# Low parts of the first network's inner activations moved from GpSimd to VectorE for two chunks

## The reference

```python
# 1. causal mix over 7 taps, softmaxed per head (8 heads of 24 channels)
out = einsum('hk,bskhg->bshg', softmax(weight), windows_of_7(x))
# 2. first network, d_ff = 1536
g = x @ w_gate;  val = x @ w_val
x = (g * sigmoid(g) * val) @ w_out
# 3. second network, d_ff = 2048
h = x @ w_in
x = where(h > 0, h, exp(min(h, 0)) - 1) @ w_out
```

## Time and profile before

| | |
|---|---|
| median of 3 runs | 1205.99 us |
| the profiled execution | 1206.76 us |
| its span, first to last instruction | 1205.0 us |
| TensorE busy | 1199.5 us, 100% |
| VectorE / ScalarE / GpSimd busy | 775.5 / 664.2 / 717.9 us |
| stages: chunk 0 first network | 13.93 to 51.05 us |
| chunk 1 first network, second network | 51.05 to 90.14, 90.14 to 124.39 us |
| chunk 2 first network, second network | 124.39 to 165.73, 165.73 to 198.52 us |

### The profile page before, as it was taken

One profiled execution on the slowest core, in us unless ns is written; L12 is line 12 of the kernel. 1 busy time (PEld: TensorE's weight loads), 2 busy tenths in 40 slices (PEclk: granted clock), 3 DMA queues, 4 the chain that ended last, 5 costly groups with the idle time before them and its releaser, 6 DMA issues.

```text
span 1205.0 us, 31390 instructions
## 1 busy us (share of the span) xinstructions
PE 1199.5 (100%) x11798; PEld 1032.4 (86%) x11798; DVE 775.5 (64%) x1178; ACT 664.2 (55%) x1114; POOL 717.9 (60%) x528
## 2 busy tenths in 40 slices
PE   9999999999999999999999999999999999999999
PEld 7988888888888888889888898888988889888898
DVE  6787575675656756567665666656666476675665
ACT  6456555465554645546455464655546556465565
POOL 6787656574654746547465474654746557465565
PEclk9999999999999999999999999999999999999999
DMA  7412012120111211012110121100212002120110
GB/s 179 109 51 44 12 27 41 32 44 11 32 31 30 44 30 23 21 30 44 30 27 17 30 44 30 35 17 22 44 30 41 11 22 44 30 44 9 30 34 15
DMA packets 103955, 43.37 MB, mean 36 GB/s; under 512 B 75888, under 2 KB 93936, under 8 KB 103920
## 3 DMA queue, kind: packets, MB, share of 16 engines
q1 hardware_dynamic: 103104, 42.29, 15.7%
q10 hardware_dynamic: 816, 0.59, 0.2%
HBM read 16.12 MB, written 6.29 MB: 19 GB/s over the span
## 4 chain that ended last, share of the span: by engine, by line
PE 97%; POOL 1%; DVE 1%; issue 1%; ACT 0%; ACTq 0%; DVEq 0%
PE up L860 55%; PE down L860 42%; POOL hid_lo L441 1%; DVE mixed L830 0%; DVE act L771 0%; PE down L1063 0%; POOL up_w_lo L326 0%; DVE hidden L787 0%; ACT L617 0%; ACT hid_hi L608 0%; POOL y_main L445 0%; POOL halves L445 0%; DVE mixed L827 0%; DVE taps_head L813 0%; ACT act L593 0%
## 5 line engine op out<-in xcount | busy, mean ns | idle before, releaser
L441 POOL TENSOR_TENSOR hid_lo<-hidden,hid_hi 128x512 fp32r<-128x512 f32 x447 | 623.7, 1405 | 473.2 <-ACT hid_hi L574 304.8
L860 PE MATMUL down<-out_w,hid_hi 64*128 64x384 f32 x2040 | 300.4, 355 | 0.0
L734 DVE TENSOR_TENSOR hidden<-act,up 128x512 f32<-128x512 f32 x191 | 130.8, 685 | 249.1 <-ACT act L557 249.1
L860 PE MATMUL down<-out_w,hid_lo 64*128 64x192 f32 x2040 | 260.8, 251 | 0.3 <-POOL hid_lo L441 0.3
L771 DVE TENSOR_SCALAR act<-up 128x512 f32<-128x512 f32 x256 | 164.8, 685 | 112.0 <-PE up L860 112.0
L860 PE MATMUL up<-in_b_hi,up_w_hi 64*128 64x512 f32 x1128 | 224.1, 393 | 0.0
L860 PE MATMUL up<-in_b_hi,up_w_lo 64*128 64x512 f32 x1128 | 223.7, 393 | 0.0
L860 PE MATMUL up<-in_b_lo,up_w_hi 64*128 64x512 f32 x1128 | 223.6, 393 | 0.0
L574 ACT ACTIVATE hid_hi<-hidden 128x512 fp32r<-128x512 f32 x192 | 121.5, 633 | 177.9 <-DVE hidden L734 160.5
L608 ACT ACTIVATE hid_hi<-hidden 128x512 fp32r<-128x512 f32 x256 | 156.9, 628 | 96.5 <-DVE hidden L787 79.4
L593 ACT ACTIVATE act<-act 128x512 f32<-128x512 f32 x256 | 156.1, 631 | 94.8 <-DVE act L771 94.8
(11 more groups left out here) (96 smaller groups left out, 1085.9 us busy)
## 6 DMA issues: line engine op xcount, KB each, us to landing
x_raw<-x_dram SPq DMA_DIRECT2D x136, 64.0 KB, 2.2
out_dram<-stage SPq DMA_DIRECT2D x15, 384.0 KB, 2.7
in_b_hi<-in_b_hi SPq DMA_DIRECT2D x32, 128.0 KB, 2.3
in_b_lo<-in_b_lo SPq DMA_DIRECT2D x32, 128.0 KB, 2.3
swapped<-halves SPq DMA_DIRECT2D x32, 128.0 KB, 2.3
in_a_hi<-in_a_hi SPq DMA_DIRECT2D x30, 128.0 KB, 2.3
in_a_lo<-in_a_lo SPq DMA_DIRECT2D x30, 128.0 KB, 2.3
stage<-w_out_dram SPq DMA_DIRECT2D x7, 384.0 KB, 3.9
```

Source lines behind the costliest of these rows:

```text
L441: return pool.tensor_tensor(hid_lo[:, slot, :], hidden[:, s, :], hid_hi[:, slot, :].bitcast(F32), ALU.subtract)
L734: v.tensor_tensor(hidden[:, f % 2, :], act[:, f % 2, :], val_bank(f, n)[:, :], ALU.mult)\
L860: return nc.tensor.matmul(dst, lhsT, rhs, start=start, stop=stop, skip_group_check=True)
```

## The change

VectorE makes the low parts of the inner activations in the first network of chunks 0 and 1 (24 of them), each one block after its product, behind the product of the next block. GpSimd makes no such low part there any more, and doesn't follow the blocks: it goes through its weight pieces, and in chunk 1 the two sums and the fold, each as soon as its inputs are there. From `elu_phase(1)` on GpSimd makes the low parts as before.

All 18 weight pieces are GpSimd's, and one semaphore counts them. The eight pieces of the second network are all handled in the first network of chunk 1, beside blocks 0, 1, 4, 5, 7, 8, 9 and 10, and none in its second network; before, five were handled there (beside 0, 1, 9, 10, 11) and three in the second network. Piece 5 moves from block 1 to block 2 of chunk 0.

In chunk 0 VectorE's transposes of the next chunk, the halo and the taps come one block later: transposes in block 2, taps in blocks 3 to 9 in place of 2 to 8. In chunk 1 the taps stay in blocks 3 to 9.

```diff
-        BESIDE0 = {1: 5, 3: 6, 5: 7, 7: 8, 8: 9}
-        BESIDE1 = {0: 10, 1: 11, 9: 12, 10: 13, 11: 14}
-        BESIDE_ELU1 = {3: 15, 4: 16, 5: 17}
+        BESIDE0 = {2: 5, 3: 6, 5: 7, 7: 8, 8: 9}
+        BESIDE1 = {0: 10, 1: 11, 4: 12, 5: 13, 7: 14, 8: 15, 9: 16, 10: 17}
+        BESIDE_ELU1 = {}
...
         def wait_weights(eng, upto):
             eng.wait_ge(piece_hi, upto)
-            for who, made in (("dve", piece_lo_dve), ("pool", piece_lo_pool)):
-                if lo_count(upto, who):
-                    eng.wait_ge(made, lo_count(upto, who))
+            eng.wait_ge(piece_lo, lo_count(upto))
...
             def mix_phase(n, extra=lambda f: None):          # GpSimd
                 for f in range(N1):
-                    pool.wait_ge(hi1_done, N1 * n + f + 1)
-                    lo_of(f % 2, f % RING).then_inc(lo1_done, 1)
+                    if is_int(n, 0) or is_int(n, 1):
+                        extra(f)
+                    else:
+                        pool.wait_ge(hi1_done, N1 * n + f + 1)
+                        lo_of(f % 2, f % RING).then_inc(lo1_done, 1)
...
-                    extra(f)
...
+            def inner_lo(n, f):                              # VectorE
+                v.wait_ge(hi1_done, N1 * n + f + 1)
+                v.tensor_tensor(hid_lo[:, f % RING, :], hidden[:, f % 2, :], hid_hi[:, f % RING, :].bitcast(F32),
+                                ALU.subtract).then_inc(lo1_done, 1)
+
             def mix_phase(n):
                 lead = isinstance(n, int)
+                own_lo = lead and n < 2
...
                     v.tensor_tensor(hidden[:, f % 2, :], act[:, f % 2, :], val_bank(f, n)[:, :], ALU.mult)\
                         .then_inc(mul_done, 1)
+                    if own_lo and f >= 1:
+                        inner_lo(n, f - 1)
...
-                    if f == 1 and is_int(n, 0):
+                    if f == 2 and is_int(n, 0):
                         transpose_x(1, 0)
                         transpose_x(1, 1)
...
-                    at = 2 if is_int(n, 0) else 3
-                    if f == at - 1:
+                    if f == 2:
                         mix(n + 1, 0)
-                    if at <= f < at + TAPS:
-                        mix(n + 1, 2 * (f - at) + 1)
-                        mix(n + 1, 2 * (f - at) + 2)
-                    if f == at + TAPS:
+                    if 3 <= f < 3 + TAPS:
+                        mix(n + 1, 2 * (f - 3) + 1)
+                        mix(n + 1, 2 * (f - 3) + 2)
+                    if f == (9 if is_int(n, 0) else 10):
                         mix(n + 1, MIX - 1)
...
+                if own_lo:
+                    inner_lo(n, N1 - 1)
```

More of the change, by code:

```diff
@@ L191, in mix_ffn_ffn @@
         piece_hi = sem("piece_hi")
-        piece_lo_dve = sem("piece_lo_dve")
-        piece_lo_pool = sem("piece_lo_pool")
+        piece_lo = sem("piece_lo")
         gate_ready = sem("gate_ready")
@@ L243, in mix_ffn_ffn, with up1_piece @@
         pieces = []
-        def up1_piece(g, who):
+        def up1_piece(g):
             c0, c1 = GROUPS[g]
@@ L249, in up1_piece, with up2_piece @@
             hi, lo = up1_w["hi"][:, :, c0:c1], up1_w["lo"][:, :, c0:c1]
-            pieces.append((loads, [(hi, s)], [(lo, s, hi)], who))
-        def up2_piece(j0, j1, who):
+            pieces.append((loads, [(hi, s)], [(lo, s, hi)]))
+        def up2_piece(j0, j1):
             s = stage[:, len(pieces) % STAGES, 0:PARTS * (j1 - j0) * P].rearrange("p (g c) -> p g c", g=PARTS)
@@ L256, in up2_piece, with out_piece @@
             hi, lo = up2_w["hi"][:, :, j0 * P:j1 * P], up2_w["lo"][:, :, j0 * P:j1 * P]
-            pieces.append((loads, [(hi, s)], [(lo, s, hi)], who))
-        def out_piece(rows, dst, q, order, who):
+            pieces.append((loads, [(hi, s)], [(lo, s, hi)]))
+        def out_piece(rows, dst, q, order):
             s = stage[:, len(pieces) % STAGES, 0:OT * D].rearrange("p (f d) -> p f d", d=D)
@@ L263, in out_piece @@
             los = [(t[:, :, to:to + n], s[:, :, of:of + n], t[:, :, of:of + n]) for to, of, n in order]
-            pieces.append((loads, [(t[:, :, 0:D], s)], los, who))
+            pieces.append((loads, [(t[:, :, 0:D], s)], los))
         def out1_piece(q):
-            out_piece(wo1_rows, out1_w, q, [(D, P, TAIL), (D + TAIL, 0, P)], "pool")
+            out_piece(wo1_rows, out1_w, q, [(D, P, TAIL), (D + TAIL, 0, P)])
         UP1_AT, OUT1_AT = {}, {}
-        for what, at, who in (("up", 0, "pool"), ("up", 1, "pool"), ("up", 2, "pool"), ("out", 0, "pool"),
-                              ("up", 3, "pool"), ("up", 4, "pool"), ("out", 1, "pool"), ("up", 5, "pool"),
-                              ("up", 6, "pool"), ("out", 2, "pool")):
+        for what, at in (("up", 0), ("up", 1), ("up", 2), ("out", 0),
+                         ("up", 3), ("up", 4), ("out", 1), ("up", 5), ("up", 6), ("out", 2)):
             if what == "up":
-                up1_piece(at, who)
+                up1_piece(at)
                 UP1_AT[GROUPS[at][0] // P] = len(pieces)
@@ L281, in mix_ffn_ffn @@
         UP2_AT, OUT2_AT = {}, {}
-        for what, at, who in (("up", 0, "pool"), ("up", 2, "pool"), ("out", 0, "pool"), ("up", 4, "pool"),
-                              ("out", 1, "pool"), ("up", 6, "pool"), ("out", 2, "dve"), ("out", 3, "pool")):
+        for what, at in (("up", 0), ("up", 2), ("out", 0), ("up", 4),
+                         ("out", 1), ("up", 6), ("out", 2), ("out", 3)):
             if what == "up":
-                up2_piece(at, at + 2, who)
+                up2_piece(at, at + 2)
                 UP2_AT[at] = len(pieces)
             else:
-                out_piece(wo2_rows, out2_w, at, [(D, 0, D)], who)
+                out_piece(wo2_rows, out2_w, at, [(D, 0, D)])
                 OUT2_AT[at * OT] = len(pieces)
         AHEAD, READY = 6, 5
-        BESIDE0 = {1: 5, 3: 6, 5: 7, 7: 8, 8: 9}
-        BESIDE1 = {0: 10, 1: 11, 9: 12, 10: 13, 11: 14}
-        BESIDE_ELU1 = {3: 15, 4: 16, 5: 17}
+        BESIDE0 = {2: 5, 3: 6, 5: 7, 7: 8, 8: 9}
+        BESIDE1 = {0: 10, 1: 11, 4: 12, 5: 13, 7: 14, 8: 15, 9: 16, 10: 17}
+        BESIDE_ELU1 = {}
         assert READY + len(BESIDE0) == PIECES1
@@ L299, in beside, with lo_count @@
             return lambda at: make(table[at]) if at in table else None
-        def lo_count(upto, who):
-            return sum(len(p[2]) for p in pieces[:upto] if p[3] == who)
+        def lo_count(upto):
+            return sum(len(p[2]) for p in pieces[:upto])
         def wait_weights(eng, upto):
             eng.wait_ge(piece_hi, upto)
-            for who, made in (("dve", piece_lo_dve), ("pool", piece_lo_pool)):
-                if lo_count(upto, who):
-                    eng.wait_ge(made, lo_count(upto, who))
+            eng.wait_ge(piece_lo, lo_count(upto))
         def stage_full(i):
@@ L319, in make_hi, with make_lo @@
                 nc.scalar.activation(dst, src, ACT.Copy).then_inc(piece_hi, 1)
[L321 to L324, removed]
+        def make_lo(pool, i):
+            pool.wait_ge(piece_hi, i + 1)
             for dst, src, hi in pieces[i][2]:
-                ins = eng.tensor_tensor(dst, src, hi.bitcast(F32), ALU.subtract)
-                ins.then_inc(piece_lo_dve if who == "dve" else piece_lo_pool, 1)
+                pool.tensor_tensor(dst, src, hi.bitcast(F32), ALU.subtract).then_inc(piece_lo, 1)
         def store_tokens(eng, m, blocks=slice(0, BLOCKS)):
@@ L490, in _ @@
             for i in range(READY):
-                make_lo(pool, i, "pool")
-            lo = lambda i: make_lo(pool, i, "pool")
+                make_lo(pool, i)
+            lo = lambda i: make_lo(pool, i)
             mix_phase(0, beside(BESIDE0, lo))
@@ L729, in mix_phase @@
                         v.wait_ge(lo1_done, N1 * n + f - 1)
-                    elif not (lead and n < 2):
+                    elif not own_lo:
                         v.wait_ge(lo2_done, N2 * (n - 1) - 1 + f)
@@ L735, in mix_phase @@
                         .then_inc(mul_done, 1)
-                    if f == 1 and not (lead and n < 2):
+                    if own_lo and f >= 1:
+                        inner_lo(n, f - 1)
+                    if f == 1 and not own_lo:
                         add_z(n - 2)
-                    if f == 1 and is_int(n, 0):
+                    if f == 2 and is_int(n, 0):
                         transpose_x(1, 0)
@@ L843, in _ @@
             mix_phase(1)
-            elu_phase(1, beside(BESIDE_ELU1, lambda i: make_lo(v, i, "dve")))
+            elu_phase(1)
             mix_phase(2)
```

## The result

| | before | after |
|---|---|---|
| median of the first comparison (8 runs each) | 1205.95 us | 1209.49 us |
| lowest and highest | 1204.83, 1207.34 | 1209.03, 1210.80 |
| ratio, 95% interval | | 1.0032 [1.0021, 1.0042] |
| second comparison (a1_again below) | 1206.29 | 1209.60, ratio 1.0025 [1.0016, 1.0034] |
| profiled execution, its span | 1206.76, 1205.0 | 1210.80, 1209.1 |

The change makes the kernel 3.3 to 3.5 us slower. Forecast were 1207.0 us and no measurable difference, with 1209.2 as the upper end of the range; both were missed.

The account below looks back on a forecast made before the run. TensorE was taken as the bound, 97% of the chain of waits. The terms -1.46 - 0.35 + 2.8 gave +1.0 us: 1207.8 from the profiled execution, 1207.0 against the median; range 1204.5 to 1209.2.

Parts of the forecast that it names:

- Bounds and stages: TensorE bounds the kernel; the change acts only before 124.39 us, and at most 1.81 us can be won.
- Part 1: Second network of chunk 1: taking the weight pieces out ends TensorE's stall, minus 1.46 us.
- stall not cured: Rival: the second network's own beat, not the pieces, causes its 1.46 us loss; 1208.5 us, chance 0.05.
- Part 2: Start of chunk 0: piece 5 one block later removes the pause before the first down-projection, minus 0.35 us.
- Part 3, chunk 0: Low parts added to VectorE in chunk 0's first network make nothing late: cost 0, bounds 0 and 0.8 us.
- Part 3, chunk 1: Chunk 1's first network: GpSimd's pieces and fold hold VectorE, so TensorE waits; plus 2.8 us, bounds 0 and 7.2.
- before projection 11 (product 9 late): Chunk 1, first network: product 9 ends at 86.3, projection 11 is due at 85.4; 0.8 us stall.
- low part 9, start of the second network: Chunk 1: low part 9, held by piece 16, ends at 91.1, due at 90.2; 0.9 us stall.
- halo copy and in_a_lo: End of chunk 1's first network: piece 17 holds the halo copy, in_a_lo ends at 93.4, due at 92.3; 1.1 us.
- the walk: Lead-in stepped forward by operation durations, VectorE waiting for GpSimd on SBUF; in chunk 1 VectorE ends 1.9 us over.
- slower: Rival: GpSimd keeps the interface across three back-to-back pairs in chunk 1; 1209.2 us, 1208.4 to 1211.4, chance 0.14.
- cover holds: Rival: chunk 1's lateness stays within 2.9 us of slack, stalls 0 to 1.4; 1204.2 to 1205.6 us, chance 0.28.

Follow-up runs that it names:

- a1_again: The changed kernel, unaltered, measured and profiled a second time: 1209.60 us against 1206.29 before, ratio 1.0025.
- e8: The kernel before with pieces 12 to 17 spread over both networks of chunk 1, piece 16 on GpSimd, no low parts moved: 1206.46 us, ratio 1.0002.
- e7: The changed kernel with GpSimd's subtractions for pieces 12 to 17 cut to the first 8 of each run of columns: 1205.96 us, ratio 0.9999.
- e5: The changed kernel with GpSimd's fold issued at block 3 of chunk 1 in place of block 6: 1209.88 us, ratio 1.0034.
- b1: The changed kernel with pieces 12 to 17 spread over both networks of chunk 1, low parts still on VectorE: 1205.51 us, ratio 0.9996.
- e2: The changed kernel with pieces 12 to 17 back at their old places, all on GpSimd, low parts still on VectorE: 1206.48 us, ratio 0.9998.

## Why the prediction was wrong

**Bounds and stages: right.** All of it lies before chunk 2; the stage there is 41.34 us in both.

**Part 1, -1.46: right in its cause (pieces in this stage), 0.17 too large.** TensorE's lateness against the kernel before falls from 5.22 to 3.93 us over this stage (3.48 to 2.19 in a1_again): 1.29. The difference is the cut that mixed a chain's time with a timeline's. The rival "stall not cured" fell, by e8 above all.

**Part 2, -0.35: right in its cause, too large.** The pause of the earlier trace rows stood in the weight loads, and there it is gone in both profiles of the change. The first down-projection starts 0.20 us earlier in a1_again than before, first the row of before:
```profile
22.59 0.96 PE L860 MATMUL down<-hid_hi,out_w 64*128 64x512 f32 x6
```
```profile
22.39 0.87 PE L865 MATMUL down<-hid_hi,out_w 64*128 64x512 f32 x6
```
What stays of it by the end of chunk 0 is 0.17 us after and 0.31 in a1_again. I had set down the whole difference of two stages as one pause.

**Part 3, chunk 0, cost 0: right.** Product 9 at 43.1 (forecast 43.2), the low parts of the input in 1.29 us from 47.60 (3.48 in the earlier trace rows), product 10 at 48.81 (forecast: ending at 49.6), no wait.

**Part 3, chunk 1, +2.8: the step that failed.** In a1_again it is 3.79. This is the term of the sum that was too small, and in it the price of piece 13 and the fold. By its three terms, from TensorE's starts against the kernel before:

| | forecast | a1_again |
|---|---|---|
| before projection 11 (product 9 late) | 0.8 | 1.62 |
| low part 9, start of the second network | 0.9 | 0.94 |
| halo copy and in_a_lo | 1.1 | 1.22 |

(The starts differ by -0.31 before, +0.83 at projection 8, +1.31 at projection 11, +2.25 at the first projection of the second network and +3.47 at the start of its step 1.) The last two terms held. The first was short by 0.82. Up to product 4 the walk was right (67.47 in the first profile, 67.3 forecast). Then it let a tap of block 5 go first, had piece 13 slip in behind it for 1.5 us, and charged 0.3 for "the fold right behind": 1.8. On the chip piece 13 was first by 0.03 us, the fold followed without a gap, and the two taps took 4.06 us, 1.40 when free: 2.66 held. Product 6 then came at 76.25, and TensorE waited at projection 8 for 1.0 us, where none was forecast. The rival "slower" named this pair and this mechanism, with a chance of 0.14; for the other two pairs it was wrong, as they didn't come back to back (0.96 us between 14 and 15, 0.36 between 16 and 17). The measured time lies in that rival's case, 1208.4 to 1211.4, but it got there with one pair of its three and with the scatter told of below: for the number that was luck. The first rival, "cover holds", fell: product 9 ended at 87.0 and 87.2 in the two profiles, not before 85.4.

The Trainium skill has the lock in SBUF — State Buffer, "SBUF: two separate sides": the operation that starts first keeps the shared ports for its whole length, and the other side blocks fully. The trace agrees (4.06 and 3.00 us for two taps). What GpSimd's subtractions of pieces 12 to 17 were worth here e7 shows: 3.5 us.

**The clock: not in the forecast at all.** In the first profile it is 1.56 us, 5.35 against 3.79 for the same matmuls; in a1_again nothing. How often it falls without a profile to show it isn't known.

**Sum.** -1.29 - 0.31 + 3.79 = +2.19 us, TensorE's distance to the kernel before from chunk 2 on in a1_again (the spans are 1205.0 and 1207.3). The medians differ by 3.3 to 3.5. The profiled execution of before was 0.77 above its median, that of a1_again 0.37 below its own, together 1.1: the rest is the scatter of single executions. Of the 102 spans of the kernel before, 15 are at 1203.4 us or below, 52 at 1203.7 to 1204.6 and 35 above; the profiled one, 1205.0, is of the highest group, while that of a1_again, 1207.3, is the third lowest of 11. What makes the groups stays open. The forecast took 0.77 off for this, set its sum on the median and gave it no width. Of the 2.5 us that the number was off, 1.2 are the terms above (0.82 of them piece 13 and the fold), and the rest is this: 1207.0 plus 1.19 would still have been 1208.2, inside the range.

## What to carry to other kernels

Where VectorE has no slack, count the pieces of GpSimd on SBUF that stand beside it, each with its whole length, and back to back ones with the length of both; moving one from a neighbour to the next doesn't change the sum (e5), only spacing them or placing them where VectorE is idle does (b1, e8). The twelve subtractions moved to VectorE in chunk 1 were nearly free here (0.17 us with the pieces early, none with them late); the placing of the weight pieces was nearly the whole difference. Take a second profile before a difference of 1 to 2 us is put down to the code.

## What the runs showed of the hardware

A small copy is held as well. The halo copy of 12 columns takes 0.16 us alone in e2, and 1.80 beside piece 17:
```profile
87.37 0.16 DVE L669 COPY halos<-x_t 128x12 f32<-128x12 f32 x1
```
The clock fell to 0.50 behind two waits of 0.57 and 0.98 us in one profile and stayed at 1.00 behind the same waits (0.57, 0.97) in another. The Trainium skill, TensorE: Matmul & The Clock Gate, "What's actually happening", says that the gate isn't tied to the kernel's start and so acts differently from run to run; these two profiles agree.

TensorE's first matmuls have two paces. Before and b1_spread, the same instructions, ahead of anything that was changed, the clock at 1.00 from 4 to 8 us in both:
```profile
5.30 1.97 PE L1063 MATMUL down<-ident,stage 128*128 128x128 f32 x8
```
```profile
5.11 1.10 PE L1068 MATMUL down<-ident,stage 128*128 128x128 f32 x8
```
The first projection starts at 13.93 and 12.86. What sets the pace isn't shown. Two of 14 profiles (b1_spread and e7) have the fast start, and 1.07 us of the scatter of times may be this; so gains of a microsecond were read from stages here, not from times.
